# Weight remainders as identity products on TensorE, the recurrence chained one group at a time, and norms and joins placed anew

## What is computed

```
# attention: normalise a, then the recurrence over t
mag = sqrt(a_re^2 + a_im^2);  a_n = a * min(mag, 0.999) / (mag + 1e-6)
S_re, S_im = a_n * S (complex);  S_re += outer(k[t], v[t]);  y[t] = q[t] @ S_re
# dense layer
h = maximum(maximum(x @ w1, x @ w2), x @ w3);  x2 = h @ w_out        # 384 -> 768 -> 384
# routed layer: each token goes to the one of 8 experts with the largest cosine
out = gate * (relu(x2 @ w1[e]) @ w2[e])                              # 384 -> 1024 -> 384
```

## Time and profile before

| | us |
|---|---|
| median of 3 runs | 1024.53 (1023.41 to 1025.75) |
| the profiled execution | 1025.89 |
| its span, first to last instruction | 1024.0 |
| DVE busy in it | 649.9 |
| PE busy | 858.9 |
| POOL busy | 481.0 |
| ACT busy | 450.2 |

### The profile page before, as it was taken

One profiled execution on the slowest core, in us unless ns is written; L12 is line 12 of the kernel. 1 busy time (PEld: TensorE's weight loads), 2 busy tenths in 40 slices (PEclk: granted clock), 3 DMA queues, 4 the chain that ended last, 5 costly groups with the idle time before them and its releaser, 6 DMA issues.

```text
span 1024.0 us, 18210 instructions
## 1 busy us (share of the span) xinstructions
PE 858.9 (84%) x6326; PEld 770.8 (75%) x6327; DVE 649.9 (63%) x1050; ACT 450.2 (44%) x834; POOL 481.0 (47%) x868
## 2 busy tenths in 40 slices
PE   1236576779898989979998999956999999999995
PEld 1235475678787878868897889856888888888885
DVE  5998866897797888849556665237522352546722
ACT  5751563555555545533444333222422342445621
POOL 1168988996089939963992000004221222323321
PEclk9556887889998999989999999985999999999998
DMA  9104144415233241403211111142711132415410
GB/s 297 57 19 120 51 100 112 113 65 150 77 91 92 74 98 52 102 32 85 62 37 44 37 37 38 63 176 74 278 43 34 46 121 79 157 43 171 152 38 31
DMA packets 42245, 90.78 MB, mean 89 GB/s; under 512 B 6312, under 2 KB 23728, under 8 KB 40768
## 3 DMA queue, kind: packets, MB, share of 16 engines
q1 hardware_dynamic: 38080, 77.48, 24.9%
q0 software_dynamic: 4096, 12.40, 3.8%
HBM read 70.20 MB, written 18.48 MB: 87 GB/s over the span
## 4 chain that ended last, share of the span: by engine, by line
PE 45%; POOL 23%; DVE 16%; issue 5%; DMA 5%; ACT 4%; SPq 1%; ACTq 0%; DVEq 0%; POOLq 0%
POOL c_re L1817 7%; POOL c_im L1818 6%; POOL ring L1820 5%; POOL ring L1821 5%; PE mm L1511 5%; PE yu L1511 4%; PE tr L1511 4%; PE mm L1515 4%; PE tr L1515 4%; PE tr L1512 4%; PE mm L1512 4%; PE yu L1512 4%; PE yu L1515 4%; PE mm L1736 3%; DMA ring<-an_scratch 2%
## 5 line engine op out<-in xcount | busy, mean ns | idle before, releaser
L1511 PE MATMUL mm<-up_hi,x_hi 128*128 128x384 f32 x432 | 162.0, 375 | 64.6 <-DVE h_sb L1064 45.7
L1512 PE MATMUL mm<-up_lo,x_hi 128*128 128x384 f32 x432 | 150.8, 349 | 0.0
L1511 PEld LDWEIGHTS mm<-up_hi,x_hi 128*128 128x128 f32 x432 | 84.8, 196 | 81.8 <-DVE h_sb L1064 51.5
L1817 POOL TENSOR_TENSOR c_re<-ring 112x128 f32<-112x128 f32 (+1 forms) x160 | 106.3, 665 | 67.8 <-DMA ring<-an_scratch 43.8
L1904 POOL DMA_INDIRECT out_rows<-g_o,rows_out x30 | 34.7, 1158 | 184.0 <-DVE g_o L1445 184.0
L900 ACT ACTIVATE g_h<-tr 128x512 f32<-128x512 f32 x60 | 35.9, 598 | 171.2 <-PE tr L1515 149.1
L1064 DVE TENSOR_TENSOR h_sb<-mm,h_sb 128x384 f32<-128x384 f32 x96 | 53.1, 553 | 85.3 <-PE mm L1515 83.1
L1818 POOL TENSOR_TENSOR c_im<-ring 112x128 f32<-112x128 f32 (+1 forms) x160 | 103.4, 647 | 0.0
L1515 PE MATMUL mm<-up_hi,x_lo 128*128 128x384 f32 x432 | 103.2, 349 | 0.0
L1820 POOL TENSOR_TENSOR ring<-c_re,c_im 112x64 f32<-112x64 f32 (+1 forms) x160 | 84.1, 526 | 12.5
L1512 PEld LDWEIGHTS mm<-up_lo,x_hi 128*128 128x128 f32 x432 | 85.4, 198 | 0.0
(11 more groups left out here) (223 smaller groups left out, 1998.4 us busy)
## 6 DMA issues: line engine op xcount, KB each, us to landing
raw<-in_moe_w SPq DMA_DIRECT2D x16, 1536.0 KB, 9.0
a_dn<-in_a_laid SPq DMA_DIRECT2D x20, 384.0 KB, 7.4
an_scratch<-a_dn SPq DMA_DIRECT2D x20, 384.0 KB, 2.3
ring<-an_scratch SPq DMA_DIRECT2D x20, 384.0 KB, 5.6
q_in<-in_q_laid SPq DMA_DIRECT2D x24, 224.0 KB, 3.0
k_in<-in_k_laid SPq DMA_DIRECT2D x24, 224.0 KB, 3.2
v_in<-in_v_laid SPq DMA_DIRECT2D x24, 192.0 KB, 3.3
x_scratch<-x_sb SPq DMA_DIRECT2D x24, 192.0 KB, 2.4
```

Source lines behind the costliest of these rows:

```text
L1511: nc.tensor.matmul(out, hi[:, x, :], w_hi(x), start=(x == 0), stop=False)
L1512: nc.tensor.matmul(out, hi[:, x, :], w_lo(x), start=False, stop=False)
L1817: nc.gpsimd.tensor_tensor(c_re[:, 0:count, :, :], cur, bc(prev[:, :, 0, :], 2, 2), ALU.mult).then_inc(chain_prod, 1)
```

## The change

1. **Low parts on PE and ACT.** There are 24 blocks: 18 of the up weights (128 x 384) and 6 of the down weights (128 x 392). For each, PE makes two products into one bank: the float32 identity with the raw weights, and `minus` (a new float32r tile, the negated identity, made by ACT) with the high part. ACT copies the bank into the low part. DVE's four subtractions are gone. On PE blocks 0 and 1 stand ahead of `router_product(0)`, 2 and 3 ahead of `router_product(1)`, 4 to 11 behind the router; in n = 0 stand 12 and 13 behind `keys_back`, 14 and 15 ahead of `answers`, and 16 to 23 behind it. On ACT the first twelve copies stand in three places ahead of the loop; in n = 0 two stand ahead of `z_recip`, two ahead of `norm_rsqrt`, and eight (16 to 23) behind `y_copy`.
2. **One group at a time.** SINGLE is gone: every group from 2 on is chained in four blocks of 16 (15 steps, 3 joins). From group 3 on POOL runs 12 steps, then `turns` of the group before, then 3 steps.
3. **Joins spread.** Group g is joined in n = 2g-2: for g = 2 to 4 the first join ahead of `z_norm`, the second behind `k_decay`, the third behind `moe_max(n-1, 1, 1)`. From g = 5 on the first stands behind `k_decay` of n = 2g-3, the second ahead of `z_norm` and the third behind `k_decay` of n = 2g-2. All of `norm_inverse` comes behind the first late join.
4. **Norms and ring loads.** n = 0, 1 and 3 make two norms, the others one, up to n = 16. Groups are loaded in n = 1, 2, 4, 5, 7, 9, 11, 13, 15, 17 (before: 1, 2, 3, 4, 5, 7, 9, 11, 13, 15).
5. **Ahead of the loop** DVE does `norm_sum` of norms 2 and 3 before the seven joins of group 0, and `norm_inverse` and `norm_apply` of both before `z_newton(0)`.

```diff
-SINGLE = 6
+        minus = sb("minus", [P, P], F32R)
...
-        def norms_in(n):
-            if n < 5:
-                return (2 * n + 4, 2 * n + 5)
-            return (n + 9,) if n + 9 < NORMS else ()
+        def norms_in(n):
+            first = 2 * n + 4 if n < 2 else n + 6 if n < 4 else n + 7
+            count = 2 if n in (0, 1, 3) else 1
+            return tuple(m for m in range(first, first + count) if m < NORMS)
...
-        ring_at = {max(g - 1, 2 * g - 7): g for g in range(DIRECT, NG)}
+        ring_at = {(g - 1 if g < 4 else 4 if g == 4 else 2 * g - 5): g for g in range(DIRECT, NG)}
...
+            def low_copy(numbers):
+                for i in numbers:
+                    _, _, lo, bank = low_block(i)
+                    act.wait_ge(lo_done, i + 1)
+                    nc.scalar.activation(lo, bank, ACT.Copy).then_inc(lo_copied, 1)
...
-            def up_low(x):
-                dve.wait_ge(up_split, x + 1)
-                nc.vector.tensor_tensor(flat(up_lo[:, x, :, :]), flat(up_raw[:, x, :, :]), flat(up_hi[:, x, :, :]).bitcast(F32), ALU.subtract) \
...
+                    wait(pe, lo_copied, i - 3 if i < 12 else i - 1)
+                    nc.tensor.matmul(bank, ident[:, :], raw, start=True, stop=False)
+                    nc.tensor.matmul(bank, minus[:, :], hi, start=False, stop=True).then_inc(lo_done, 1)
...
-            for g in range(SINGLE, NG, 2):
-                if g > SINGLE:
-                    turns(g - 2)
-                chain_steps(g, range(1, 17))
-                turns(g - 1)
-                chain_steps(g, range(17, HALF // 2))
+            for g in range(DIRECT + 1, NG):
+                chain_steps(g, range(1, 13))
+                turns(g - 1)
+                chain_steps(g, range(13, BLK))
```

More of the change, by code:

```diff
@@ L449, in chain_of @@
                 return ring_8[:, g, :, :, :, :]
-            if g < SINGLE:
-                return ring_b[:, g % RING, :, :, :, :]
-            return ring_q[:, g // 2 % 2, :, :, :, :]
+            return ring_b[:, g % RING, :, :, :, :]
         def steps_of(g):
             return list(chain_of(g).shape)[2] - 1
-        chains = [g for g in range(1, NG) if g < SINGLE or g % 2 == 0]
         def steps_before(g):
-            return sum(steps_of(c) for c in chains if c < g)
+            return sum(steps_of(c) for c in range(1, g))
         def joins_of(g):
@@ L824, in _ @@
                     kp_copy(n)
+                if n == 0:
+                    low_copy(range(12, 14))
                 if more and late_z:
@@ L831, in _ @@
                     norm_mag(m, norm_of(m))
+                if n == 0:
+                    low_copy(range(14, 16))
                 for m in norms:
@@ L837, in _ @@
                     y_copy(n)
+                if n == 0:
+                    low_copy(range(16, LOWS))
                 if prev:
@@ L1181, in _ @@
                 ending = norms_in(n - 1) if 1 <= n <= NC else ()
-                late = joins_late.get(n)
-                apart = 0 if n in (2, 10) else 1
+                late = joins_late.get(n, ())
                 if prev2:
@@ L1202, in _ @@
                     norm_m2(m, norm_of(m))
-                if n in joins_early:
-                    for number in range(len(joins_of(joins_early[n]))):
-                        join(joins_early[n], number)
-                if n == 0:
-                    up_low(1)
+                for g, number in joins_early.get(n, ()):
+                    join(g, number)
                 if more:
                     z_norm(n + 1)
-                if n == 0:
-                    up_low(2)
-                if late is not None:
-                    for number in range(apart):
-                        join(late, number)
                 if prev:
@@ L1227, in _ @@
                     k_decay(n + 1)
+                for g, number in late[:1]:
+                    join(g, number)
                 for m in norms:
                     norm_inverse(m, norm_of(m))
-                if late is not None:
-                    for number in range(apart, len(joins_of(late))):
-                        join(late, number)
+                if prev:
+                    moe_max(n - 1, 1, 1)
+                for g, number in late[1:]:
+                    join(g, number)
                 if more:
                     rotation(n + 1)
-                if prev:
-                    moe_max(n - 1, 1, 1)
-                if n == 1:
-                    dve.wait_ge(dn_split, 1)
-                    nc.vector.tensor_tensor(flat(dn_lo[:, :, :]), flat(dn_raw[:, :, :]), flat(dn_hi[:, :, :]).bitcast(F32), ALU.subtract).then_inc(dn_split, 1)
                 if n == NC - 2:
@@ L1638, in _ @@
                 if now:
+                    if n == 1:
+                        pe.wait_ge(lo_copied, LOWS)
                     keys_back(n)
+                if n == 0:
+                    low_parts(range(12, 14))
                 if prev:
@@ L1646, in _ @@
                 if now:
+                    if n == 0:
+                        low_parts(range(14, 16))
                     answers(n)
+                if n == 0:
+                    low_parts(range(16, LOWS))
                 if prev:
```

96 lines of the change are left out of this document (61 added, 35 removed).

## The result

The changed kernel takes 995.25 us (median of four, 994.66 to 996.5), the kernel before in the same comparison 1024.4 (1023.41 to 1025.75). The ratio is 0.9716, with a 95% interval of 0.9699 to 0.9733. The forecast was 993.5 in a range of 981 to 1021. The profiled execution of the changed kernel took 995.13 us, its span is 993.4.

What follows compares the result with a forecast made beforehand. PE's pace of 21.61 us a chunk was the floor, with losses above it mainly from DVE's joins and norms and waits for POOL. Terms 2 - 13 - 26 + 6 = -31 us gave 993.5 us, range 981 to 1021.

Steps and rivals of the forecast that it cites:

- part 1: Low parts moved from DVE to PE and ACT; all but the shift of z_norm(3) was held swallowed ahead of it.
- Term A: Start of z_norm(3), set by the end of group 2's chain plus a join: 129 to 142, +2 us (-4 to +9).
- Term B: One norm fewer in iterations 2 and 4, two back in 15 and 16: -13 us (0 to -17).
- Term C: From 254.19 us on, single chains and spread joins can remove all loss over PE's pace: -26 us.
- D: DVE late from more joins, in even iterations 8 to 16 and odd ones: +6 us taken, +4 to +33 possible.
- with a join in its own place each time: Condition, with chains ending one group at a time, for all 26.0 us lost from 254.19 on to go.
- The start eats half: Rival at the start: low clock, 1.6 us blocks, late PE and ACT, chains holding early iterations; 1009.5 us, chance 0.17.
- DVE full: Rival in the iterations with added joins: DVE's lateness at its upper end, +33, giving 1020.5 us; chance 0.09.
- POOL becomes the bound: Rival in the chains of groups 4 to 11: steps above 2.9 us set the pace, 1046.5 at 3.3; chance 0.12.
- none over 25: Sign: no step between ACT's copies of chunks 4 to 17 should exceed 25 us.
- 21.6 to 22.5: Sign: ACT's copies of chunks 4 to 17 should stand 21.6 to 22.5 us apart.
- an even iteration longer than 24: Sign against: the prediction is wrong if even iterations are longer than 24 us.

Runs made afterwards that it cites:

- the run with less load on DVE: The changed kernel with the last join of each of groups 5 to 11 cut to 4 of its 16 columns: 988.2 us, ratio 0.9637.
- the run with group 3 spread: The changed kernel with all joins of group 2 behind k_decay and group 3's joins spread over iterations 3 and 4: 993.45 us, ratio 0.968.

## Why the prediction came out right

The sum was -31 us on the span, and -30.6 came. By place, though, two errors of about 6 us cancel, and that the forecast came so close is luck. The terms gave -11 up to chunk 3 and -20 behind it; measured were -17.0 and -14.4 (and +0.8 behind chunk 17).

**The low parts.** A block cost 1.60 us at the low clock, the upper end of my 1.0 to 1.6, and not the 1.3 that I took. Taking 0.32 us off it for the float32r product leaves 1.28 for the float32 one, four times 0.32. The Trainium skill (FP8 and Floating Point Precision, TensorE Precision Notes) gives a true float32 product four passes through the array, and the trace agrees. The size did not matter: chunk 0's scores came 5.9 us later (3 to 8 predicted), `x_hi` came at 87.39 (88 predicted), the joins of group 1 at 93.47 (95), chain 2 at 101.20 (102). But the reason given for the last of these times, eight blocks and their copies ahead of `x_hi`, is only half of it. They do stand there, yet with all blocks taken out and the new order ahead of the loop kept, `x_hi` was at 86.66 and chain 2 at 101.30. That order alone brings these times, and the prediction had no term for it there. "All else of part 1 ... is swallowed by it" was nearly right. Three subtractions are; the fourth, which stands beside chain 2, costs 3 us, in part by the very effect of the earlier trace rows that I had used only for POOL's mean step.

**Term A** (the start of `z_norm(3)`, +2, likeliest 135, range 129 to 142): it came at 137.91, 5.0 later than before. The new wait ahead of it costs 4.2 us in all, as the run without it shows (995.25 less 991.05). I had reckoned the place rightly and named the cause, the early join. But the sum carried A to every copy, and chunk 0's copy does not wait for `z_norm(3)`: it stands ahead of it. Instead of 2 later it came 4.5 earlier, because one norm fewer in iteration 2 gives 5.2 us back there. These 6.5 us are the error of the first part.

**Term B** (fewer norms early, -13): the norms are worth 12.2 us at chunk 3, so the size was right, but not the place. Term B was written for the stretch from chunk 0 to 3, and the norms give only 6.9 of the 12.5 us won there (92.05 us with the old norms, 85.13 without). The other 5.6 (97.61 to 92.05) come with the old norms too. No term of the prediction held them. The joins of groups 2 and 3 stand elsewhere in this stretch, but no run isolates them. A term is missing as well: the changed kernel takes 2.6 us longer from chunk 4 to 17 than with the old norms, 1.5 of it where the two norms now stand. I had set that at nothing, by 9.6 us of room in the earlier trace rows, but joins stand there too.

**Term C** (-26, everything over PE's pace from chunk 4 to 17 can go) **with D** (+6): -20 was written, -14.4 came. For the twelve steps from chunk 5 on, D's +6 is near: 6.6 over the pace. What failed is the sentence "with a join in its own place each time". Group 4's joins all stand in iteration 6, two of them late, beside a norm; D counted the iterations 8 to 16 only. That step is 26.65 us, 5.0 over the pace, and the step of iteration 7, not counted either, is 1.2 over it. Reading the table of joins for g < 5 would have given most of it: 17.14 + 3 x 2.63 = 25.0.

**The even and the odd steps.** 0.8 us over the pace was written for the even ones, 0.75 to 1.2 came (22.36 to 22.84 us), and the run with less load on DVE shows the cause. For the odd ones nothing, or at the worst 2.0, was written; of those from iteration 9 on, two are at the pace and three are 0.5 to 0.6 over it.

**The rivals.** "The start eats half" wanted A at +9 and B at -4; 5.0 and 12.2 came. The blocks did cost 1.60 us at the low clock, but the clock rose over large parts of the start, as the point against this rival had it. "DVE full" is what happens by its mechanism, but at another price: all that is over the pace from chunk 4 to 17 is 11.7 us, where this rival had 33. "POOL becomes the bound" did not come: the mean step is 0.675 + 0.674 + 0.529 + 0.557 = 2.44 us, under the 2.6 named, and no join from group 6 on waits for POOL. Its four lines on the page:

```profile
L1857 POOL TENSOR_TENSOR c_re<-ring 112x128 f32<-112x128 f32 (+1 forms) x157 | 106.0, 675 | 77.7 <-DMA ring<-an_scratch 62.0
L1858 POOL TENSOR_TENSOR c_im<-ring 112x128 f32<-112x128 f32 (+1 forms) x157 | 105.9, 674 | 0.0
L1860 POOL TENSOR_TENSOR ring<-c_re,c_im 112x64 f32<-112x64 f32 (+1 forms) x157 | 83.0, 529 | 12.3
L1861 POOL TENSOR_TENSOR ring<-c_re,c_im 112x64 f32<-112x64 f32 (+1 forms) x157 | 87.5, 557 | 0.0
```

POOL even waits for the ring's load before eight of the ten groups (62.0 us in all, 43.3 of it before groups 2 and 4, and 2.1 to 4.0 before each from group 7 on). So from there on the chains follow the loads and not POOL's own pace.

**The signs I named.** Wrong: "none over 25" (26.65) and "21.6 to 22.5" (20.22 to 22.84 in the other steps). By my own words an even iteration longer than 24 would make the prediction wrong. From chunk 4 on there is one, iteration 6 (ahead of it iterations 2 and 4 are longer too), and the total came so close only because the start gave more. Right: chunks 0 to 3 at 85.1 for 84 (but see term B), chunk 0's copy before 145, waits for POOL only in iteration 2, apart from 0.50 us before group 5's first join.

## What to carry to other kernels

When an engine that runs in order is nearly full, reckon its work step by step from the tables that place it, for every iteration, the first ones too; a wait that shows behind a full engine is a symptom, and moving what is waited for brings nothing until load goes. An operation placed so that it waits for a chain on another engine can cost its wait and whatever lengthens that chain, so look for work that is ready and can stand ahead of it; the run with group 3 spread shows that taking a join forward into such a wait loses again. Here, chaining one group at a time was worth only what it let one spread.

## What the runs showed of the hardware

PE's granted clock at the start followed what the change put there: 0.66 from 60 to 70 us for 0.50 before, and the page's second part has it in the first four fortieths of the span at 9, 8, 7 and 8 tenths, where the page of before has 9, 5, 5 and 6. The runs show that it is the added blocks. With the low parts back on DVE these four read 9, 5, 5 and 6 again, and 60 to 70 us is at 0.50; the kernel before with the low parts alone has 9, 8, 7 and 8, and 0.69.

A subtraction of 2.59 us on DVE with two operands in SBUF held one POOL instruction for 3.15 us where its like takes as little as 0.32. The row of POOL's instruction begins at 122.93, while DVE's operation before the subtraction, which also has two operands, still runs, and ends 0.2 us behind the subtraction. The Trainium skill states (SBUF — State Buffer, SBUF: two separate sides) that the one of the two engines that starts first keeps the shared ports for its whole instruction and the other is blocked. The rows agree, if POOL's instruction was held over two DVE operations in a row. The operations of 112 x 384 added on DVE show the same from the other side. Where POOL's instruction of 0.46 us had begun just before (303.36 us, DVE's at 303.49), DVE's took 0.74; where DVE's began first (394.11, POOL's at 394.25), it took 0.54 and POOL's 0.71. New to me was the price: not the mean of many steps, but up to 3 us of the kernel's time, because this one chain was awaited.
